# Attention and two routed expert layers on one core: reordering the seams between the stages

## The reference

```python
for t in range(S):                       # r, k, v, w: [4, 8, 768, 48]
    kt, vt, rt, wt = (k[:, :, t], v[:, :, t], r[:, :, t], w[:, :, t])
    cur = einsum('bhd,bhe->bhde', u[None] * kt, vt)
    y[:, :, t] = einsum('bhd,bhde->bhe', rt, state + cur)
    state = wt[..., None] * state + einsum('bhd,bhe->bhde', kt, vt)

# layer 1: x [3072, 384], w1 [8, 384, 1024], w2 [8, 1024, 384]
logits = (x / |x|) @ (emb / |emb|).T / tau
expert_idx = argmax(logits); probs = softmax(logits)
out[mask] = gate_w[mask, None] * (relu(x[mask] @ w1[e]) @ w2[e])     # for each expert e

# layer 2: the same with logits = x @ w_gate, and a second gate
out[mask] = gate_w * sigmoid(x @ w_output_gate)[mask, e] * (relu(x[mask] @ w1[e]) @ w2[e])
```

## Time and profile before

| | us |
|---|---|
| three runs | 788.15, 793.58, 794.45 |
| median | 793.58 |
| the profiled execution | 787.61 |
| its span, first to last instruction | 785.9 |
| attention, to about | 165 |
| seam to layer 1 | 165 to 203 |
| layer 1, loop over its tiles | 203 to 481 |
| seam to layer 2 | 481 to 511 |
| layer 2, loop over its tiles | 511 to 770 |

### The profile page before, as it was taken

How to read it: one execution, slowest core, us unless ns; L and a number is a source line. 1 busy time by engine, 2 the same in 40 slices (tenths; PEclk the granted TensorE clock), 3 DMA queues, 4 the chain that set the end, 5 groups by cost and what they waited for, 6 DMA issues and landing times.

```text
span 785.9 us, 20353 instructions
## 1 busy us (share of the span) xinstructions
PE 726.7 (92%) x5566; PEld 646.2 (82%) x5567; DVE 502.6 (64%) x1359; ACT 389.8 (50%) x761; POOL 159.8 (20%) x202
## 2 busy tenths in 40 slices
PE   2998898983999999999999998799999999999993
PEld 2787777763899999999999997699999999999993
DVE  7999999996567665847667674464444445336521
ACT  3666777781546454536456463154343535245421
POOL 5445566553000000000000001000111000000000
PEclk9999999996999999999999999899999999999998
DMA  6666688625735251505253351353333333316110
GB/s 135 155 156 157 183 261 244 161 95 176 271 106 168 94 170 40 192 28 172 85 169 119 120 184 37 119 195 108 133 110 120 124 125 113 120 35 196 40 35 27
DMA packets 50268, 103.75 MB, mean 132 GB/s; under 512 B 7921, under 2 KB 29904, under 8 KB 50224
## 3 DMA queue, kind: packets, MB, share of 16 engines
q1 hardware_dynamic: 29536, 67.18, 27.1%
q10 hardware_dynamic: 15568, 21.76, 10.3%
q0 software_dynamic: 5120, 14.26, 5.0%
HBM read 85.73 MB, written 19.01 MB: 133 GB/s over the span
## 4 chain that ended last, share of the span: by engine, by line
PE 76%; DVE 13%; issue 5%; DMA 2%; POOL 1%; ACT 1%; DVEq 0%; POOLq 0%; SPq 0%; ACTq 0%
PE bank L1320 20%; PE bank L1346 20%; PE bank L1354 10%; PE bank L1325 10%; PE bank L1335 6%; DVE SF L773 3%; DVE Q L764 3%; PE bank L1309 2%; PE bank L1287 2%; DVE Kb L778 1%; PE bank L1280 1%; DVE dv L783 1%; DVE YT L816 1%; PE bank L1136 1%; PE bank L1201 1%
## 5 line engine op out<-in xcount | busy, mean ns | idle before, releaser
L1320 PE MATMUL bank<-wall,xT_hi 128*128 (+1 forms) x660 | 180.0, 408 | 1.3 <-ACT xT_hi L655 1.3
L1346 PE MATMUL bank<-wall,hT_hi 128*128 x880 | 164.9, 338 | 0.5 <-ACT hT_hi L664 0.5
L1346 PEld LDWEIGHTS bank<-wall,hT_hi 128*128 128x128 f32 x880 | 153.0, 188 | 3.1 <-issue 0.7
L1320 PEld LDWEIGHTS bank<-wall,xT_hi 128*128 128x128 f32 x660 | 119.1, 191 | 22.0 <-issue 1.8
L879 DVE TENSOR_TENSOR wall<-raw,wall 128x1024 f32 (+1 forms) x96 | 112.0, 1221 | 31.3 <-ACT wall L561 28.2
L659 ACT ACTIVATE hs<-bank 128x512 f32<-128x512 f32 x110 | 65.3, 594 | 129.6 <-PE bank L1325 129.6
L1038 DVE TENSOR_TENSOR xT_lo<-bank,xT_hi 128x384 fp32r<-128x384 f32 x57 | 31.8, 558 | 107.4 <-ACT xT_hi L655 107.4
L561 ACT ACTIVATE wall<-raw 128x1024 f32 (+1 forms) x96 | 95.0, 1051 | 10.4 <-issue 10.4
L1325 PE MATMUL bank<-wall,xT_lo 128*128 (+1 forms) x330 | 94.9, 396 | 0.0
L664 ACT ACTIVATE hT_hi<-bank 128x512 fp32r<-128x512 f32 x110 | 59.9, 596 | 68.6 <-PE bank L1335 68.6
L1354 PE MATMUL bank<-wall,hT_lo 128*128 x440 | 91.2, 349 | 0.0
(11 more groups left out here) (196 smaller groups left out, 983.4 us busy)
## 6 DMA issues: line engine op xcount, KB each, us to landing
raw<-wall_in SPq DMA_DIRECT2D x96, 512.0 KB, 3.8
xin<-sorted ACTq DMA_DIRECT2D x59, 194.0 KB
rk<-rk_in SPq DMA_DIRECT2D x46, 192.0 KB
v_in<-v_src ACTq DMA_DIRECT2D x24, 192.0 KB
vT<-vT_in ACTq DMA_DIRECT2D x48, 96.0 KB
wb<-w_in SPq DMA_DIRECT2D x46, 96.0 KB
sorted<-padrow SPq DMA_DIRECT2D x16, 194.0 KB, 2.0
sorted<-yrow,slot POOLq DMA_INDIRECT x28, 2.6
```

The costliest lines, as they stand in the source:

```text
L1320: pe.matmul(bank[n][:, :], xT_hi[:, k, :], w[:, bass.ds(slot, 1), cols].rearrange("p o n -> p (o n)"), start=(k == 0 and w is w_hi), stop= ...
L1346: pe.matmul(bank[2][:, 0:DM], hT_hi[:, j, :], w[:, bass.ds(slot, 1), W2 + j * DM:W2 + (j + 1) * DM].rearrange("p o n -> p (o n)"), start=( ...
```

## The change

Six edits, none of which changes what is computed:

1. `place1` is split. `gates1`, the sum of the softmax and its reciprocal, now stands ahead of the flag; in the last chunk the slots are written before the totals are summed and cast into `padi`; and VectorE reads the flag back only after `tables(0)`.
2. `pads` takes a list of experts. In the first layer SyncE pads experts 0 and 1, waits for tile 0 (`x_in` 16) and pads 2 to 7. In both layers ScalarE loads tile 1 after the pads of experts 0 and 1, and tile 2 after all.
3. VectorE splits the LATE pieces of expert 0 behind `rest_xt(0)` and no longer ahead of the layer.
4. The last row tile of layer 1 has its own buffers `yrow_last` and `slot2_last`, filled by `keep_last_row` and `place_last_row`, which has one instruction less; `n_e` is worked out behind it.
5. GpSimd issues the last scatter of each layer behind its loop, the one of layer 1 without a wait for the scatter before.
6. In `gated`, the copies of the token stand ahead of the wait for the second product.

```diff
@@ block.sync
-            def pads(m):
+            def pads(m, experts):
                 sp.wait_ge(padaddr[m], 1)
-                for e in range(E):
+                for e in experts:
                     row = sp.value_load(padi[0:1, m, e:e + 1], ...)
-                    sp.dma_start(...).then_inc(pads_done[m] if e else pad0_done[m], 16)
+                    sp.dma_start(...).then_inc((pad0_done[m], pad1_done[m], pads_done[m])[min(e, 2)], 16)
...
-            pads(0)
+            pads(0, range(2))
+            sp.wait_ge(moes[0]["x_in"], 16)
+            pads(0, range(2, E))
             sp.wait_ge(moes[0]["x_in"], 32)
             for k in range(RAWS, 2 * E * RAWS):
                 if k == (E + 2) * RAWS:
-                    pads(1)
+                    pads(1, range(E))
@@ block.gpsimd
-            with gp.Fori(0, last + 2) as p:
+            with gp.Fori(0, last + 1) as p:
                 gp.wait_ge(rts[1]["slots"], p + 2)
+                scatter_row(slot2, yrow)
                 gp.wait_ge(moes[0]["sc"], 16 * p + 16)
                 gp.sem_inc(row_free, 1)
+            gp.wait_ge(rts[1]["slots"], last + 3)
+            scatter_row(slot2_last, yrow_last)
...
-            with gp.Fori(0, last + 1) as p:
+            with gp.Fori(0, last) as p:
                 gp.wait_ge(mo["y_sb"], p + 2)
+                scatter_out()
                 gp.wait_ge(mo["sc"], 16 * p + 16)
                 gp.sem_inc(mo["y_free"], 1)
+            gp.wait_ge(mo["y_sb"], last + 2)
+            scatter_out()
+            gp.wait_ge(mo["sc"], 16 * last + 16)
@@ block.scalar
+            def keep_last_row(g):
+                act.wait_ge(moes[0]["y_sb"], g)
+                act.activation(yrow_last[:, 0:DM], ybuf[:, :], ACT.Copy).then_inc(rts[1]["row"], 1)
...
-                act.wait_ge(pads_done[m], 16 * E - 16)
+                act.wait_ge(pad1_done[m], 16)
                 load_rows(1)
                 for n in range(2):
                     relu(0, n)
                 copy_xt(1)
+                act.wait_ge(pads_done[m], 16 * E - 32)
                 load_rows(2)
...
-                    keep_row(last + 2)
+                    keep_last_row(last + 2)
@@ block.vector
-            def place1(n, c, q):
-                den, at = r4[:, 9, :], r4[:, 1, :]
+            def gates1(n, q):
+                den = r4[:, 9, :]
                 ...
                 step1(n, 10, v.reduce_sum(den, z4[:, 1], AXX))
                 step1(n, 11, v.tensor_scalar(den, den, 1e-9, None, ALU.add))
                 v.reciprocal(rows[:, q, :, GATE], den)
+            def place1(n, q):
+                at = r4[:, 1, :]
+                last = n % NCHUNK == NCHUNK - 1
                 v.wait_ge(rt["cnt"], n + 1)
-                if n % NCHUNK == NCHUNK - 1:
-                    v.reduce_sum(sum8[:, :], TOTALS.rearrange("p (b e) -> p e b", e=E), AXX)
                 v.tensor_tensor(z4[:, 2], RANKS..., oh5[:, n % 2, 1:], ALU.mult)\
-                 .then_inc(rt["rread"], 1)
+                 .then_inc(rt["ranked" if last else "rread"], 1)
                 v.reduce_sum(placed[:, :], oh5[:, n % 2]..., AXX).then_inc(rt["base"], 1)
-                v.wait_ge(rt["rread"], n + 1)
-                if n % NCHUNK == NCHUNK - 1:
-                    v.tensor_copy(padi[:, 0, :], sum8[:, :]).then_inc(padaddr[0], 1)
+                if last:
+                    v.wait_ge(rt["ranked"], n // NCHUNK + 1)
+                else:
+                    v.wait_ge(rt["rread"], n + 1)
                 step1(n, 12, v.reduce_sum(at, z4[:, 2], AXX))
                 v.tensor_copy(slot4[:, q], at).then_inc(rt["slots"], 1)
+                if last:
+                    v.reduce_sum(sum8[:, :], TOTALS..., AXX).then_inc(rt["rread"], 1)
+                    v.wait_ge(rt["rread"], n + 1)
+                    v.tensor_copy(padi[:, 0, :], sum8[:, :]).then_inc(padaddr[0], 1)
...
             choose1(LC)
+            gates1(LC, LC % 2)
             v.wait_ge(fl_ps, 1)
             link(v.tensor_scalar(flagp[0:1, 3:4], ...))
             v.tensor_scalar(flag[0:1, 0:1], ...).then_inc(fl_ready, 1)
+            place1(LC, LC % 2)
+            counts1(link)
+            tables(0, link)
             v.wait_ge(fl_ready, 1)
             bad = v.value_load(flag[0:1, 0:1], min_val=0, max_val=1)
-            place1(LC, LC, LC % 2)
-            counts1(link)
-            tables(0, link)
             with v.If(bad > 0):
...
+            def place_last_row(g):
+                v.wait_ge(r2["cnt"], g)
+                step(4, v.scalar_tensor_tensor(..., accum_out=slotf))
+                v.tensor_scalar(slot2_last[:, :], slotf, t10, None, ALU.add)
+                v.tensor_copy(yrow_last[:, TOK:TOK + 1], ytok)
+                v.wait_ge(r2["ex"], g)
+                step(5, v.tensor_scalar(ex, ex, 1.0, None, ALU.add))
+                step(6, v.tensor_scalar(sec, se, 1e-9, ex, ALU.add, ALU.mult))
+                v.reciprocal(yrow_last[:, GATE:GATE + 1], sec).then_inc(r2["slots"], 1)
...
-            for q in LATE:
-                split_lo(0, 0, q)
             link(v.memset(ybuf[:, :], 0.0))
             link(v.memset(yrow[:, :], 0.0))
+            link(v.memset(yrow_last[:, DM:], 0.0))
...
                 def gated(g):
-                    v.wait_ge(mo["mm2"], g + 3)
                     ...                                    # copies of the token
+                    v.wait_ge(mo["mm2"], g + 3)
                     v.tensor_scalar(ybuf[:, :], bank[2][:, 0:DM], gate, None, ALU.mult).then_inc(mo["y_sb"], 1)
...
                 keep_ext(0)
                 rest_xt(0)
+                if m == 0:
+                    for q in LATE:
+                        split_lo(0, 0, q)
                 keep_ext(1)
                 rest_xt(1)
...
                     v.tensor_copy(padi[:, 1, :], bank[3][:, 48:48 + E]).then_inc(padaddr[1], 1)
+                    place_last_row(last + 2)
                     link(v.tensor_tensor(n_e, bank[3][:, 48:48 + E], ecap[:, :], ALU.subtract))
-                    place_row(last + 2)
                     tables(1, link)
```

More of the change, by code:

```diff
@@ L195, in build @@
         pads_done = [sem(f"pads_done{m}") for m in range(2)]
+        pad1_done = [sem(f"pad1_done{m}") for m in range(2)]
         pad0_done = [sem(f"pad0_done{m}") for m in range(2)]
@@ L460, in _, with scatter_row @@
             last = gp.value_load(tab[0:1, 0, TAB_LAST:TAB_LAST + 1], min_val=E - 1, max_val=TILES - 2)
-            with gp.Fori(0, last + 2) as p:
-                gp.wait_ge(rts[1]["slots"], p + 2)
+            def scatter_row(slot, row):
                 part(gp)
                 gp.indirect_dma_start(
-                    out=sorted2, out_offset=bass.IndirectOffsetOnAxis(ap=slot2[:, :].bitcast(U32), axis=0),
-                    in_=yrow[:, :], in_offset=None, bounds_check=SLOTS - 1, oob_is_err=False)\
+                    out=sorted2, out_offset=bass.IndirectOffsetOnAxis(ap=slot[:, :].bitcast(U32), axis=0),
+                    in_=row[:, :], in_offset=None, bounds_check=SLOTS - 1, oob_is_err=False)\
                   .then_inc(moes[0]["sc"], 16)
+            with gp.Fori(0, last + 1) as p:
+                gp.wait_ge(rts[1]["slots"], p + 2)
+                scatter_row(slot2, yrow)
                 gp.wait_ge(moes[0]["sc"], 16 * p + 16)
                 gp.sem_inc(row_free, 1)
+            gp.wait_ge(rts[1]["slots"], last + 3)
+            scatter_row(slot2_last, yrow_last)
             mo = moes[1]
```

21 lines of the change are left out of this document (16 added, 5 removed).

## The result

| | before | changed |
|---|---|---|
| median of six runs each, side by side | 793.18 us | 787.91 us |
| lowest to highest | 788.15 to 795.01 | 786.71 to 788.85 |
| profiled execution (its span) | 787.61 (785.9) | 788.66 (786.9) |
| a second measurement, medians (34 and 12 runs) | 791.55 | 790.04 |

The ratio is 0.9943, with an interval of 0.9916 to 0.997: 0.6% faster, within the 1% that was called no change. In the second measurement the changed kernel gave 0.9974 (0.995 to 0.9999). The two intervals share the stretch from 0.995 to 0.997, which is 2.4 to 4.0 us.

A forecast was written before the change was run, and what follows sets the result against it. TensorE bounds the expert loops, so only two seams and the end can gain: 2.0 + 3.4 + 0.2 = 5.6 us, taking the profiled 787.61 to 782.0 and the median 793.58 to 788.0; range 783.0 to 792.5.

The forecast's parts named there:

- The slots: First seam, VectorE: moving the flag's read and softmax sum, and taking totals off the chain, brings the scatters 1.3 us earlier.
- The landing of the last scatter: First seam: with two pads ahead instead of eight, the last scatter lands in 2.6 us, not 4.7; 2.1 us gained.
- TensorE's side: First seam: tile 0 transposed 2.3 us earlier, first product at full clock 1.8 us shorter; 4.1 us on TensorE's own side.
- Raw pieces are late next: First seam: ScalarE waits for expert 1's raw weight pieces, TensorE idles about 2 us before the router's product; gain only 2.0.
- The wait of tile 2 for six pads: First seam: ScalarE waits for six pads before loading tile 2, delaying the copies of hT; costs nothing, raw pieces being later.
- Late splits at no cost: First seam, VectorE: three late splits, 3.50 us, go behind xT_lo of tile 0; all that waits is later, nothing paid.
- The second seam: Between the expert layers: 0.6 us from the chain, 1.0 from tile 1's earlier load, 1.8 from full clock; 3.4 in all.
- The clock falls: Rival: clock drops in the 2 us gap before the router's product or in the second seam; gain 3.9, 789.7; chance 0.25.
- Raw in time: Rival, first seam: raw weight pieces arrive in time, so TensorE's side gives its 4.1; gain 7.7 us, 785.9; chance 0.12.
- slower: Rival, first seam: raw pieces land slowly, the third at 210.2, and the clock falls; 1.0 us slower, 794.6; chance 0.05.
- Landing unchanged: Rival, first seam: last scatter still takes 4.7 us because four scatters queue on one another; first seam gives 0, 790.0; chance 0.08.
- GpSimd paid nothing at its loop's exit: Rival: GpSimd's last scatters, now behind the loops, pay 0.9 us at each loop's exit; gain 3.8, 789.8; chance 0.08.

The follow-up runs named there:

- before again: The kernel before, with no edit, measured and profiled once more: 791.71 us, ratio 0.9993.

## Why the forecast was right, and where its steps were not

*The median.* 788.0 was forecast and 787.91 measured, and that closeness is luck. The seams and the end gave 3 to 3.6 us, not the 5.6 of the sum; of 793 this is a ratio of 0.9955 to 0.9962, which lies in the intervals of both measurements. The other 2 us of the first measurement are most likely chance: the kernel before had a median of 793.18 in six runs, and of 791.5 to 791.6 in three larger measurements of 31 to 34, and the changed kernel had 790.04 in the second. The single execution, for which the sum gave 782.0, took 788.66: 4.8 of the difference is attention, and the rest the sum.

*The slots,* 1.3: right, 1.31 (7.60 to 6.29).

*The landing of the last scatter,* 4.7 to 2.6: mis-sized. It took 3.4. The step took the chunk before as the same transfer without pads. The runs with one pad and none (3.6) show that pads make 1.3 of the difference and that 0.7 to 1.0 have another cause. What that is stays open: the four scatters follow one another at 1.29 us in both chunks, and no run changed anything else about them.

*TensorE's side:* the transpose of tile 0 went from 14.98 behind the one-hot to 13.43 in the profiled execution and 12.93 in the other, 1.6 and 2.1 where 2.3 was forecast. Warming took 6.23 us in the former, not 5.50. The first product kept the clock, as forecast, but so did that of before again, behind a gap of 1.68, so the 1.8 us is no effect of the change and the gap did not decide it.

*Raw pieces are late next:* for the changed kernel the mechanism is as forecast, down to the 1.9 us of idle time ahead of the router's product. The size was off, 2.0 against 0.7 (0.4 by the means of three). The pieces were issued at 19.00 where the step had 18.6, since tile 0 landed 0.7 later and the six pads took 6.7, not 7.0. The third landed 7.3 us after the first issue, not 6.5. Together with 0.2 in ScalarE's copies that is 1.4 us, and it turns 2.0 into 0.6 or 0.7. Behind this lies a premise that failed: that ScalarE splits without a wait in the kernel before. That was so in the one execution that the prediction read, where the clock had fallen. At full clock the pieces set the end there too, and the change issued them only 18.63 to 19.00 behind the one-hot instead of 19.16 to 19.58.

*The wait of tile 2 for six pads,* put at nothing: the copies of hT were to be done at 22.1 behind the one-hot and were done at 23.3. The raw pieces came later still, so nothing was paid, but by 0.9 and 0.3 us only.

The estimate by the Trainium skill (DMA: Bandwidth & Descriptors, Anatomy of one DMA), which the prediction set beside its own, gave 5.6 for the third piece and is farther off from the 7.3 measured. The page fits that sum to DMAs that GpSimd issues, which the prediction does not say; these are SyncE's.

*Late splits at no cost:* right, and the 0.3 to 0.8 that their old place costs agrees with "keeps VectorE off the path".

*The second seam,* 3.4 = 0.6 + 1.0 + 1.8: the sum came out at 2.5 to 2.7, with terms that were wrong. The chain gave its 0.6 at the scatter (6.89 to 6.33). The 1.8 for the clock was worth nothing against the kernel before, because before again, at full clock, took 23.57; once tile 1 is in time a fall costs that much (22.27 against 20.57). The mistake was to add it to tile 1: both delays lie side by side, and the later one decides. Tile 1 alone was worth 1.8 to 2.2 (21.55 against 23.30 to 23.78), not 1.0.

*The end,* 0.2: right (11.29 to 11.10), half of it ahead of the last scatter's issue (1.75 to 1.64) and half behind.

*The rivals.* "The clock falls" happened in one of two executions of the changed kernel, behind the very gap that was named, at about 1.5 us; with the same first seam and a gap of 2.09 it did not (the run with tile 1's wait put back). "Raw in time" and "slower" did not. "Landing unchanged" is refuted, though part of what it named, the four scatters on one another, may be in the 0.7 to 1.0 left open. GpSimd paid nothing at its loop's exit: from the start of the last row's reciprocal, which completes the row, to the scatter are 1.04 us in the second seam of both kernels. The Trainium skill (Runtime: NRT & Kernel Launch, Instruction fetch mechanics) puts the cost on a taken branch whose target is not at hand; the loop's exit into the next lines is not one, and the trace agrees.

*Versions that do better.* All pads ahead of tile 0 (0.9933), or the raw pieces before the seam (0.9931), with the rest of the change kept. Their first seams are 0.9 to 1.7 us shorter than the changed kernel's. Their intervals overlap that of the changed kernel's first measurement and barely touch that of its second, so the seams are the evidence, not the medians.

## What to carry to other kernels

Ahead of a stretch, list every transfer that its first work needs and give each a due time; an order that speeds up the first of them by holding back the last moves the wait and may lengthen it. Two delays on the same wait, such as a low clock and a late tile, must not be added: ask what the later one would be if the other were gone. And before a sum is made on one profiled execution, its stages should be held against a second one, since a clock level or a fast attention in it may be luck. Here the one profile hid, behind a fallen clock, the wait that already ended the first seam.

## What the runs showed of the hardware

- Two executions of one kernel differ by up to 6.0 us in attention (180.11 and 186.09 to the same instruction); over all kernels of the study that point was at 180.1 to 186.1.
- The granted clock behind a short gap differed from one execution to the next. In the kernel before TensorE went to 0.50 behind gaps of 1.24 and 0.98 us, and behind 1.68 and 1.02 in the same places stayed at 1.00; in the changed kernel it fell behind 1.23 and kept the clock behind 1.86. A fall costs 1.5 to 1.8 us when nothing hides it (a loop 1.5 us longer; a second seam of 22.27 instead of 20.57; a first product of 3.84 instead of 2.07).
- What stood ahead of a DMA mattered more than its size: 194 KB landed in 2.4 us with little beside them and in 7.03 behind three loads of 512 KB. The first of a row of 512 KB pieces landed in 3.8 us, the third 6.7 to 7.6 us after the first was issued.
- Pads of 194 KB beside a scatter delay its landing only in number: 3.3 to 3.6 us with two, one or none, 4.5 to 5.1 with eight.
- VectorE's first instruction behind the branch over the redo code came after 3.19, 3.86 and 3.59 us of issue (changed kernel, and late splits back in place), the longest wait without a releaser on VectorE in this seam. In the last two the flag's read, 1.15 us before, is in it.
